# An FFT filter and two MLPs on one core: six more of the sixteen frequency units turned by quarter products

## What is computed

```
X = np.fft.rfft(x, axis=1)                   # x: (2, 3008, 256)
Y = X * (filt_r + 1j * filt_i)[None, :, :]
y = np.fft.irfft(Y, n=3008, axis=1)          # then reshaped to (6016, 256)
h = y @ w_in;   g = np.maximum(0.01 * h, h);  y = g @ w_out      # 256 -> 2048 -> 256
h = y @ w2_in;  r = np.maximum(h, 0);         out = (r * r) @ w2_out
```

## Time and profile before

| | before |
|---|---|
| median of three executions | 1063.19 us |
| profiled execution, its own time | 1064.17 us |
| its span in the profile | 1062.0 us |
| TensorE busy (matmul) | 1056.9 us, 100% |
| weight loads busy | 881.0 us, 83% |
| VectorE, ScalarE, GpSimd busy | 831.8, 561.7, 320.2 us |
| whole turns, line 991 | 80 transposes in 10 units |
| quarter turns, line 1000 | 384 matmul records in 6 units |

### The profile page before, as it was taken

How to read it: one execution, slowest core, us unless ns; L and a number is a source line. 1 busy time by engine, 2 the same in 40 slices (tenths; PEclk the granted TensorE clock), 3 DMA queues, 4 the chain that set the end, 5 groups by cost and what they waited for, 6 DMA issues and landing times.

```text
span 1062.0 us, 14667 instructions
## 1 busy us (share of the span) xinstructions
PE 1056.9 (100%) x5456; PEld 881.0 (83%) x5456; DVE 831.8 (78%) x1142; ACT 561.7 (53%) x979; POOL 320.2 (30%) x287
## 2 busy tenths in 40 slices
PE   9999999999999999999999999999999999999998
PEld 9559888888888888888998888888888888888998
DVE  2878998887887887787887886887887887786666
ACT  3666665554554655555554554544554554454543
POOL 1895764434343343341221211220220220210000
PEclk9999999999999999999999999999999999999999
DMA  9786000122112112112344000100100100100100
GB/s 313 213 280 222 10 1 18 35 53 49 49 51 48 52 48 51 52 34 54 120 152 145 21 1 1 40 1 1 40 1 1 40 1 1 40 0 1 40 1 35
DMA packets 66727, 61.48 MB, mean 58 GB/s; under 512 B 40689, under 2 KB 53857, under 8 KB 66657
## 3 DMA queue, kind: packets, MB, share of 16 engines
q1 hardware_dynamic: 66160, 60.06, 18.3%
q10 hardware_dynamic: 496, 0.49, 0.1%
HBM read 36.55 MB, written 23.99 MB: 57 GB/s over the span
## 4 chain that ended last, share of the span: by engine, by line
PE 98%; DMA 1%; DVE 0%; POOL 0%; ACT 0%; issue 0%; SPq 0%; DVEq 0%; ACTq 0%
PE PS L1092 16%; PE PS L1091 16%; PE PS L1090 16%; PE PS L1098 14%; PE PS L1100 14%; PE PS L1099 14%; PE PS L1064 2%; PE PS L964 2%; PE PS L1044 1%; PE PS L1021 1%; PE PS L991 1%; DMA X<-in_x 1%; PE PS L1000 1%; DVE GF L905 0%; POOL AF L465 0%
## 5 line engine op out<-in xcount | busy, mean ns | idle before, releaser
L709 ACT ACTIVATE GH<-GF 128x512 fp32r<-128x512 f32 (+1 forms) x384 | 238.7, 622 | 298.6 <-DVE GF L907 154.3
L913 DVE TENSOR_TENSOR GL<-GF,GH 128x512 fp32r<-128x512 f32 (+1 forms) x384 | 272.1, 712 | 109.4 <-ACT GH L709 102.6
L1092 PE MATMUL PS<-GH,WOL 128*128 128x512 f32 (+1 forms) x768 | 295.8, 385 | 0.0
L1090 PE MATMUL PS<-GH,WOH 128*128 128x512 f32 (+1 forms) x768 | 295.8, 385 | 0.0
L1091 PE MATMUL PS<-GL,WOH 128*128 128x512 f32 (+1 forms) x768 | 295.8, 385 | 0.0
L1098 PE MATMUL PS<-XH,WIH 128*128 128x512 f32 (+1 forms) x672 | 259.7, 386 | 0.3 <-ACT SN L687 0.3
L1100 PE MATMUL PS<-XH,WIL 128*128 128x512 f32 (+1 forms) x672 | 258.8, 385 | 0.0
L905 DVE SCALAR_TENSOR_TENSOR GF<-GF 128x512 f32<-128x512 f32 (+1 forms) x192 | 172.8, 940 | 1.6
L1091 PEld LDWEIGHTS PS<-GL,WOH 128*128 128x128 f32 x768 | 144.2, 188 | 27.0
L1092 PEld LDWEIGHTS PS<-GH,WOL 128*128 128x128 f32 x768 | 144.2, 188 | 26.8
L1090 PEld LDWEIGHTS PS<-GH,WOH 128*128 128x128 f32 x768 | 144.2, 188 | 26.7
(11 more groups left out here) (92 smaller groups left out, 948.4 us busy)
## 6 DMA issues: line engine op xcount, KB each, us to landing
V<-zu SPq DMA_DIRECT2D x12, 512.0 KB, 7.0
zu<-U SPq DMA_DIRECT2D x31, 192.0 KB, 3.7
out_y<-YT SPq DMA_DIRECT2D x5, 1024.0 KB, 4.3
X<-in_x SPq DMA_DIRECT2D x8, 512.0 KB, 9.5
wi<-PWH SPq DMA_DIRECT2D x16, 224.0 KB, 2.5
wi<-PWL SPq DMA_DIRECT2D x16, 224.0 KB, 3.1
WIH<-wi SPq DMA_DIRECT2D x8, 448.0 KB, 3.6
WIL<-wi SPq DMA_DIRECT2D x8, 448.0 KB, 4.4
```

Of the source, the lines that this page charges most:

```text
L709: nc.scalar.activation(GH[:, g, 0:width(s)], GF[:, g, 0:width(s)], ACT.Copy).then_inc(g_hi[kind], 1)
L913: nc.vector.tensor_tensor(GL[:, g, 0:w], GF[:, g, 0:w], GH[:, g, 0:w].bitcast(f32), ALU.subtract).then_inc(g_lo[kind], 1)
L1090: nc.tensor.matmul(acc, wh, xh, start=first, stop=False)
L1092: return nc.tensor.matmul(acc, wl, xh, start=False, stop=last)
```

## The change

The quarter form was used in the even units from 4 on (4, 6, 8, 10, 12, 14). Now it is used in all units from 4 on, so that units 5, 7, 9, 11, 13 and 15 are new.

```diff
         def by_quarters(i):
 
-            return i >= 4 and i % 2 == 0
+            return i >= 4
 
         def turned_steps(i):
```

## The result

The median of eight executions after the change is 1066.11 us, beside 1063.43 us for eight of the kernel before: a ratio of 1.0036, 95% interval 1.002 to 1.0052 (the ratios here go by the means; the medians differ by 2.68 us). The change makes the kernel some 3 us slower, where 0.8 us faster was forecast; 1066.1 lies outside the range of 1061.3 to 1063.8. The profiled execution took 1065.91 us, with a span of 1063.8.

A forecast was written before the change was run, and what follows sets the result against it. TensorE was taken as the bound: six units each 0.28 us shorter, at most 1.68, cut by data waits to a 0.80 us gain. 1063.19 - 0.80 gave a median of 1062.4 us, range 1061.3 to 1063.8.

The forecast's parts named there:

- What bounds the kernel: TensorE, busy 972.38 of 975.66 us from the last V load on, so the MLPs pass on any head start.
- The 6.43 us from spectrum to inverse as the second limit: Data take 6.43 us from a unit's spectrum to its inverse, so every third unit waits; gain 0.80 instead of 1.68.
- A unit in 2.62 on TensorE: With a quarter turn, a unit takes TensorE 2.62 us instead of 2.90, at most 1.68 us gained over six units.
- the walk: Following TensorE's inverses unit by unit, the later of TensorE and data deciding: last spectrum at 68.65 instead of 69.45.
- The price of a quarter turn is not a guess: Unit 6's quarter turn has 64 records done in 0.89 us; this price was taken for all six new ones.
- The cover of 0.15 on ScalarE: ScalarE's two copies finish 0.15 us before they would delay the next quarter turn; costed at nothing.
- Rival 3: Waiting for both ScalarE copies limits quarter turns to one per 2.90 us: 0.43 us slower, 1063.6 us; chance 0.08.
- The pause of unit 10: VectorE starts unit 10 1.70 us after its spectrum, not 1.24, with 0.77 idle unexplained; assumed to stay.
- The V loads move along: After the last spectrum, V loads and their first use shift with it, no DMA backlog holding them: near 81.5 and 85.5.
- Rival 4: Quarter turns issue at 25 ns a record, 1.60 us instead of 0.89: 4.3 us more, 1066.6 us; chance 0.01.

The follow-up runs named there:

- q57: The changed kernel with only units 5 and 7 as new quarter turns, 9, 11, 13 and 15 whole again: 1063.34 us, ratio 0.9999.
- no9_15: The changed kernel with the turns of units 9 and 15 whole again: 1063.86 us, ratio 1.0006.
- lite: The changed kernel without the filter loads of units 9 to 15 (older filters used, output differs) and with first V loads only after unit 12's store: 1072.87 us.
- again: The changed kernel run and profiled once more, unedited: 1070.0 us, ratio 1.0056.
- shift64: The changed kernel with 16 more one-column warm-up matmuls (64 TensorE instructions) at the very start: 1072.05 us, ratio 1.0083.

## Why the prediction was wrong

- **What bounds the kernel**: right. TensorE, and the MLPs pass on the head start or the delay (975.54 and 975.68 us).
- **The 6.43 us from spectrum to inverse as the second limit**: right. Inverse 3 starts 6.43 after its spectrum, and after the first pause so do inverse 8 (51.17 to 57.63, 6.46) and inverse 11 (59.59 to 66.03, 6.44).
- **A unit in 2.62 on TensorE**: right where instructions are there (40.02 to the undisturbed 42.64, and inverses 2 and 4 lie on the walk within 0.02). q57 bears the walk out to 0.01 us, no9_15 to 0.20 (single profiles).
- **"The price of a quarter turn is not a guess"**: this step failed. The 64 records in 0.89 are right, and ten of the twelve quarter turns of after have 0.89 to 1.17. But the row comes from a kernel in which a quarter turn stands in every second unit, and it was multiplied as if the supply of instructions had no rate of its own. I counted 192 matmuls for 48 transposes in time on the array and not in instructions: a unit with a quarter turn has 162 instructions and takes 2.62 us, so 256 last 4.1 us on average. From a crossing to a usable packet, counting 1.3 us behind the packet's end, the two traces show 3.5 to 6.3 us under this DMA load. Before, a stretch of 256 lasted at least 6.3, and nothing stopped; after, two packets of seven came too late, and that cost 3.5 us. The term for the supply of instructions is missing from the sum.
- **The cover of 0.15 on ScalarE "at nothing"**: right, no turn waited for line 566. Rival 3 didn't occur.
- **The pause of unit 10, taken over as it is**: it stayed. VectorE begins that unit at 58.15, 1.65 after its spectrum, again with no releaser in the profile. Before, a packet of q14 (8 KB, instructions too) lies at 57.50 to 57.93, and after one lies at 58.10 to 58.64. A fetch as on TensorE doesn't fit these two: VectorE goes on at 57.85 and 58.15, before the packet has ended, where TensorE goes on more than 1 us after the end. No run tested it, and the cause of this pause stays open.
- **The V loads move along**: right, 16.85 us for 16.89.
- **Rival 4, quarter turns issue slower**, had the right sign and some of the size, at a chance of 0.01, but another mechanism: not each record is slower, the stream stops twice. The six quarter turns that "speak against it" stood too far apart to show it.
- **The chances**: a loss of some 3 us stood only in rival 4, at 0.01, and was left out of the range, because no term of the sum could lose more than a few tenths.

What is shown: the place of the pauses follows the count of instructions, and they end a steady time after the end of an instruction packet. In the thirteen profiles of after and of the experiments, a break of over 0.2 us inside a quarter turn stands at 193 or 194 above a multiple of 256, with one exception: a break at count 1244 in turn 8 of after (0.26 from one record to the next) and of lite (0.41), which stays unexplained. A pause needs neither the quarter form nor a lower clock. What is argued: that the packet is late because of the loads and stores on the DMA engines. For it speak that in this stage no packet waited over 1.7 us while the DMA engines were nearly idle, and the single execution of lite. Why one crossing is followed by its packet after 1.1 us and another after 4.0 stays open.

## What to carry over

An edit that replaces a few long instructions by many short ones has a second price beside the engine's time: the instructions themselves. Divide 256 by the instructions per microsecond of the new stretch, and compare it with the longest way from one crossing to the next usable packet in the trace of before, in a stretch with the same DMA load; here 4.1 us stood against 6.3. This tells that a pause can come, not where or how long: no9_15 had a stretch of 3.28 us without one. Where an engine stops in the middle of a group with "issue" as the releaser, count its instructions up to there before looking for a wait.

## What the hardware did that I had not expected

- TensorE paused up to 2.62 us for its own instructions (again, turn 15: 68.63 to 71.25), while the page showed the instruction queue at 0.3%. A packet of 16 KB took 0.88 to 2.63 us, and TensorE went on 1.06 to 1.59 us after its end in 33 of 35 stops.
- A pause can cost the clock as well. In `again` the granted clock falls to the lower level (1.2 GHz) behind the pause that ends at 71.25; the windows, columns as above:

```profile
70.00:72.00 2.00, 0.74 (x8) 0.48 (x11) 0.00 (x0) 0.26 (x1) 2.00 (x2) 0.81 1.04 342
72.00:74.00 2.00, 2.00 (x13) 0.69 (x9) 0.46 (x1) 0.83 (x2) 0.01 (x1) 0.50 1.00 384
```

  It stays there until 78 us. shift64 shows the same behind its pause of 2.08 us:

```profile
73.00:74.00 1.00, 0.63 (x29) 0.62 (x32) 0.00 (x0) 0.00 (x0) 0.98 (x1) 0.79 1.03 395
74.00:75.00 1.00, 1.00 (x25) 0.57 (x20) 0.00 (x0) 0.43 (x1) 1.00 (x2) 0.50 1.00 384
```
